# A fused attention, expert and MLP kernel: VectorE makes all tables of picks, ScalarE one product of the carry, and the MLP's step 1 is put in another order

## What is computed

```python
q_bucket, k_bucket = hash_of_signs(q @ proj), hash_of_signs(k @ proj)   # 6 bits
scores = where(q_bucket == k_bucket, q @ k.T / sqrt(64), -1e9)          # 2 x 8 heads, 768 x 768
x = softmax(scores) @ v                                                 # as rows: 1536 tokens x 512

logits = x @ w_gate + modality_bias[modality_id]                        # 8 experts
e = argmax(logits); gate = softmax(logits)[e]
y = gate * (relu(x @ w1[e]) @ w2[e])                                    # 512 -> 1024 -> 512

h = y @ w_in                                                            # 512 -> 2048
out = (maximum(h, 0) + log1p(exp(-abs(h)))) @ w_out                     # 2048 -> 512
```

## Time and profile before

| | us |
|---|---|
| median of 3 runs | 731.88 (731.85 to 732.01) |
| the profiled execution | 733.24 |
| its span, first to last instruction | 731.4 |
| attention and what comes ahead | 0 to 234.8 |
| dispatch | 234.8 to 272.1 |
| expert layers | 272.1 to 460.6 |
| MLP | 460.6 to 731.4 |

### The profile page before, as it was taken

One profiled execution on the slowest core, in us unless ns is written; L12 is line 12 of the kernel. 1 busy time (PEld: TensorE's weight loads), 2 busy tenths in 40 slices (PEclk: granted clock), 3 DMA queues, 4 the chain that ended last, 5 costly groups with the idle time before them and its releaser, 6 DMA issues. The chain is left out here.

```text
span 731.4 us, 13094 instructions
## 1 busy us (share of the span) xinstructions
PE 709.6 (97%) x4028; PEld 603.5 (83%) x4028; DVE 558.1 (76%) x897; ACT 489.1 (67%) x919; POOL 328.8 (45%) x303
## 2 busy tenths in 40 slices
PE   7999999999999979999999999999999999999996
PEld 4999999999998768888888878778887888878884
DVE  8999999989997556549991262598888788887874
ACT  7888888878887545459982464666566566566562
POOL 7987886788722710000000000255545845557543
PEclk9999999999999989999999999999999999999999
DMA  4215411132063483239990000133233423234221
GB/s 136 73 40 173 164 39 58 49 118 77 19 231 115 134 289 141 92 138 343 347 378 1 0 29 0 53 94 112 86 96 93 158 96 104 86 91 168 86 77 67
DMA packets 40530, 85.05 MB, mean 116 GB/s; under 512 B 5584, under 2 KB 9840, under 8 KB 40496
## 3 DMA queue, kind: packets, MB, share of 16 engines
q1 hardware_dynamic: 37776, 77.01, 31.2%
q0 software_dynamic: 2000, 6.98, 2.9%
q10 hardware_dynamic: 720, 0.64, 0.3%
HBM read 76.82 MB, written 6.68 MB: 114 GB/s over the span
## 5 line engine op out<-in xcount | busy, mean ns | idle before, releaser
L606 POOL TENSOR_TENSOR hres<-hexp,hres 128x512 f32<-128x512 f32 x46 | 60.0, 1305 | 306.7 <-DVE hres L1338 210.3
L678 ACT ACTIVATE pTh<-psA 128x384 fp32r<-128x384 f32 x192 | 83.8, 490 | 36.2 <-PE psA L1416 34.9
L966 DVE TENSOR_TENSOR pTl<-psA,pTh 128x384 fp32r<-128x384 f32 x192 | 97.9, 552 | 11.1 <-ACT pTh L678 9.7
L959 DVE TENSOR_SCALAR_CACHE_REDUCE psA<-psA 128x768 f32<-128x768 f32 x96 | 91.8, 956 | 1.7 <-PE psA L1410 1.6
L1410 PE MATMUL psA<-K,Q 128*128 128x384 f32 x384 | 89.9, 356 | 2.5 <-ACT probs L662 1.6
L662 ACT ACTIVATE probs<-psA,negmax 128x768 f32<-128x768 f32 x96 | 87.4, 911 | 0.4 <-DVE psA L959 0.4
L877 ACT ACTIVATE habs<-psA 128x512 f32<-128x512 f32 x48 | 28.7, 598 | 77.9 <-PE psA L1689 73.9
L1244 DVE TENSOR_TENSOR wil<-rawi,wih 128x512 fp32r<-128x512 f32 x48 | 77.5, 1617 | 0.0
L609 POOL TENSOR_TENSOR hsum<-hsum,hres 128x512 f32<-128x512 f32 x46 | 69.5, 1512 | 10.1 <-POOL hres L606 8.7
L1228 DVE SCALAR_TENSOR_TENSOR hTl<-psA,hTh 128x512 fp32r<-128x512 f32 x32 | 21.8, 685 | 67.5 <-ACT hTh L783 67.5
L1717 PE MATMUL psA<-woh,sl 128*128 128x512 f32 x180 | 70.2, 390 | 0.8 <-DVE sl L1317 0.8
(11 more groups left out here) (255 smaller groups left out, 1693.6 us busy)
## 6 DMA issues: line engine op xcount, KB each, us to landing
w2s<-in_moe_w SPq DMA_DIRECT2D x9, 2048.0 KB, 8.8
w1s<-in_moe_w SPq DMA_DIRECT2D x9, 2048.0 KB, 7.8
rawi<-in_moe_w_in SPq DMA_DIRECT2D x48, 256.0 KB, 2.7
rawo<-in_moe_w_out SPq DMA_DIRECT2D x48, 256.0 KB, 2.7
raw<-in_qk SPq DMA_DIRECT2D x16, 384.0 KB, 3.1
vs<-in_v SPq DMA_DIRECT2D x16, 192.0 KB, 2.4
x_rows<-X SPq DMA_DIRECT2D x1, 1728.0 KB, 6.5
x_rows<-X SPq DMA_DIRECT2D x1, 1512.0 KB, 5.5
```

The costliest lines, as they stand in the source:

```text
L678: nc.scalar.activation(pTh[u // TPGR % 2][:, g * TPH:(g + 1) * TPH, u % TPGR * P:(u % TPGR + 1) * P], psA[2][:, g, 0:HALF].rearrange("p (t ...
L959: V.tensor_scalar(psA[u % 2][:, :, 0:HALF], psA[u % 2][:, :, 0:HALF], PENALTY, PENALTY, ALU.min, ALU.min, accum_out=negmax[:, u % 4:u % 4 ...
L966: V.tensor_tensor(pTl[u // TPGR % 2][:, g * TPH:(g + 1) * TPH, cols], psA[2][:, g, 0:HALF].rearrange("p (t n) -> p t n", t=TPH), pTh[u // ...
```

## The change

In the dispatch VectorE makes all twelve tables of picks in two instructions of six, where it made ten in two of five; GpSimd's two are gone. ScalarE makes the carry's product with the row number, behind the exponential of the gates, and GpSimd keeps the other. On TensorE one group of the early first layer is done behind the 24 products and not ahead of them. In the MLP's step 1 VectorE makes its `hsum` ahead of `sl` of step 0, and the last expert tile is taken out of PSUM behind step 3, by ScalarE and by VectorE.

```diff
-PICKED = TILES - 2
...
             pool.tensor_tensor(carry[:, :, 0, :], within[:, :, :], over(iota_t[:, 0:TILES], TILES), ALU.mult).then_inc(carry_ready, 1)
-            pool.tensor_scalar(carry[:, :, 1, :], within[:, :, :], row_of[:, :], None, ALU.mult).then_inc(carry_ready, 1)
-            pool.wait_ge(lane_ready, 1)
-            for t in range(PICKED, TILES):
-                pool.tensor_scalar(pick[:, t, :], iota_p[:, :], lane_f[:, t:t + 1], None, ALU.is_equal).then_inc(carry_ready, 1)
...
             nc.scalar.activation(tmp8[:, :, :], tmp8[:, :, :], ACT.Exp).then_inc(gexp_done, 1)
+            act.wait_ge(consts, 12)
+            act.wait_ge(within_ready, 1)
+            nc.scalar.activation(carry[:, :, 1, :], within[:, :, :], ACT.Copy, scale=row_of[:, :]).then_inc(carry_ready, 1)
...
-                    if k == 1:
+                    if k == 3:
                         high_x2(final, nc.scalar.snap(col, min_val=0, max_val=B * S))
...
             for h in range(2):
-                ts = slice(h * PICKED // 2, (h + 1) * PICKED // 2)
-                V.tensor_tensor(pick[:, ts, :], iota_p[:, :].unsqueeze(1).broadcast_to([P, PICKED // 2, P]),
+                ts = slice(h * TPB, (h + 1) * TPB)
+                V.tensor_tensor(pick[:, ts, :], iota_p[:, :].unsqueeze(1).broadcast_to([P, TPB, P]),
                                 over(lane_f[:, ts], P), ALU.is_equal).then_inc(pick_ready, 1)
...
                     split_wo(k - 1, 1 - u)
-                    low(k - 1, 1 - u)
                     dve.wait_ge(l_done, k + 1)
                     V.scalar_tensor_tensor(hsum[u][:, :], hps[u], 0.0, hlog[u][:, :], ALU.max, ALU.add).then_inc(sum_done, 1)
+                    low(k - 1, 1 - u)
                     split_wi(k + LAG, u)
...
-                    if k == 1:
+                    if k == 3:
                         low_x2(final, nc.vector.snap(col, min_val=0, max_val=B * S))
...
-            first_layer(range(2, 6), w1s[1], xT0)
+            first_layer(range(2, 5), w1s[1], xT0)
...
-                if t < PICKED:
-                    pe.wait_ge(pick_ready, 1 + t // (PICKED // 2))
-                else:
-                    pe.wait_ge(carry_ready, 3 + t - PICKED)
+                pe.wait_ge(pick_ready, 1 + t // TPB)
...
-            first_layer(range(6, FC), w1s[1], xT0)
+            first_layer(range(5, FC), w1s[1], xT0)
```

## The result

| | before | after |
|---|---|---|
| median | 732.03 (731.61 to 733.43, 16 runs) | 730.38 (728.78 to 731.46, 16 runs) |
| span of the profiled execution | 731.4 | 729.4 |
| first gather starts | 243.41 | 242.26 |
| ScalarE and VectorE released | 260.74 to 260.80 | 259.56 to 259.62 |
| first turn of a layer row behind the gathered tiles (`yrow_bits`) | 271.70 | 270.42 |

A forecast was written before the change was run, and what follows sets the result against it. TensorE, busy 445.5 of 447.0 us from 272.05 us, was taken as the bound, so time saved earlier counts. Gathers and stall -1.3 us plus MLP -0.6 us give -1.9 us: 731.88 to 730.0 us, range 726.6 to 732.2 us.

The forecast's parts named there:

- Picks: Dispatch: VectorE's tables end at 240.5 to 240.7 us; `source` and the first gather come 1.3 us earlier, at 241.15 and 242.1 us.
- The product on ScalarE: Dispatch, carry's product: takes 0.3 us, 0.6 us at most; costs nothing, up to 0.3 us on hT.
- TensorE "has work queued until 257.4 us": Dispatch: TensorE stays busy until the stall, so earlier gathers by themselves do not speed it up before then.
- two signs of being wrong: Dispatch: TensorE running out before 257 us, or gathers lengthening once VectorE's gate chain overlaps them otherwise, would refute the forecast.
- rival 3: Dispatch: late signals start at an earlier turn and two more turns fall into the stall; +2.7 us, 734.6 us; chance 0.12.
- The stall: Dispatch, TensorE's 4.21 us gap: its end hangs on the gathers' end, so -1.3 us; bounds 0 and -1.3 us.
- The clock: Behind the stall, 1.2 GHz stretch: taken as unchanged, 0 us; bounds 0 and -2.8 us if the shorter gap keeps full clock.
- The MLP: Steps 1 to 3: earlier `hsum` cuts TensorE's step 3 wait, -0.6 us; x2h and x2l in step 3 cost nothing.
- Rival 4: MLP step 1: GpSimd takes the shared port first, TensorE waits 1.4 us for sl of step 0; 731.0 us; chance 0.06.
- Rival 2: Dispatch: the stall's end doesn't move, gathers not its cause; only the MLP's 0.6 us stays, 731.3 us; chance 0.17.
- rival 1: Dispatch: the shorter gap keeps the clock full, also -2.8 us, 727.2 us; chance 0.21.
- Rival 5: Dispatch: the stall vanishes, gathers running out before TensorE gets there; 4.2 + 2.8 + 0.6 gives 724.3 us; chance 0.07.

The follow-up runs named there:

- before_again: Kernel before, unaltered, run and traced once more in a place with late signals: 732.01 us, ratio 0.9994.
- mlp_only: Kernel before with only the MLP's edits, nothing of the dispatch: 731.77 us against 732.39 us, ratio 0.9995.
- dispatch_only: Changed kernel with the MLP's edits taken back: 730.07 us, ratio 0.9968 against the kernel before.
- after_again: Changed kernel, unaltered, run and traced once more in a place with late signals: 730.25 us, ratio 0.9970 against the kernel before.
- spare13: Changed kernel plus 13 matmuls on constants in TensorE's program ahead of the turn that waits in the stall: 730.32 us, ratio 0.9969 against the kernel before.
- extra3: Changed kernel plus three gathers into scratch tiles behind the twelve: 734.2 us, ratio 1.0027 against the kernel before.
- fourbuf_again: Changed kernel with four gated-row tiles and four PSUM turn buffers, not two: 727.74 us, ratio 0.9938; as fourbuf, without late signals, 723.58 us, 0.9981.
- throttle_again: Changed kernel with at most two gathers under way: 732.13 us, ratio 0.9991 against the kernel before at 732.72 us.
- group_ahead: Changed kernel with the early first layer's sixth group back ahead of the picks, in a place without late signals: 723.61 us, ratio 0.9979 against the kernel before.

## Why the prediction was right

The traces with late signals side by side (us; the release is VectorE's last one by such a signal, near the end of the gathers; "at 1.2 GHz" is the length of the stretch, wherever it starts):

| kernel | first gather | release | at 1.2 GHz | `yrow_bits` turn | from there to the end |
|---|---|---|---|---|---|
| before | 243.41 | 260.74 | 6.8 | 271.70 | 459.7 |
| before_again | 243.34 | 260.75 | 6.8 | 270.50 | 459.8 |
| mlp_only | 243.32 | 260.45 | 6.8 | 270.74 | 459.2 |
| dispatch_only | 241.93 | 259.13 | 3.4 | 268.90 | 459.8 |
| after | 242.26 | 259.56 | 6.8 | 270.42 | 459.0 |
| after_again | 242.34 | 259.53 | 3.4 | 270.23 | 459.0 |
| spare13 | 242.21 | 259.48 | 3.4 | 270.95 | 459.2 |
| extra3 | 242.26 | 263.66 | 10.2 | 274.37 | 459.3 |
| fourbuf_again | 242.00 | 259.43 | 0 | 266.70 | 459.2 |

- **Picks.** Right: tables end at 240.68 us (240.5 to 240.7 said), `source` 241.31 us (241.15), first gather 242.26 us (242.1). Of the 1.15 us the moved group gave about 0.35 us.
- **The product on ScalarE.** 0.40 us, between the 0.3 us taken and the bound of 0.6 us; it cost nothing.
- **TensorE "has work queued until 257.4 us".** This step failed. TensorE waits 1.19 us for the gates' sum, whose signal is held. It cost only 0.25 us at the stall's start, which is why the sum still held. The prediction gave two signs of being wrong, and both came: TensorE runs out before 257 us, and a gather is longer beside VectorE. It is also the first half of rival 3: the late signals do start earlier. Its second half, that more turns fall behind the stall, didn't happen here: the turn that waits is the same.
- **The stall.** Right in cause: the release follows the gathers' end, and extra3 moves it the other way. In size -1.18 us for -1.3 us, as the first gather moved by 1.15 us and not by 1.3 us. The reason given for it was not right: "issued at a fixed rhythm" fails, since of the 1.15 us at the first gather 0.81 us are left at the last. The release keeps its distance from the first gather (17.33 us before, 17.30 us after) and not from the last instruction, which ends 2.3 us ahead of it before (258.46 us) and 1.9 us after (257.65 us). Both repeats have the same releases to 0.03 us. What the prediction left open (why a signal is late) is now narrower: with three or more gathers under way, at the rate that they then have, TensorE is held.
- **The clock.** The value taken, 0, is what the two profiled executions show (6.8 us at 1.2 GHz in both, 0.7 and 0.9 us of it in the gap); before_again and after_again show that it could have come out otherwise, so this match is luck too. The reason given for the other bound was weak. The clock fell 1.9 us after TensorE ran out here and some 3.5 us after in the earlier trace rows, so a gap of 3.1 us was no protection, and a stretch of 3.4, 6.8 or 10.2 us followed in others. This term scatters by itself, some 1.7 us for 3.4 us more or less (at half the clock, work of that length loses half): the runs of the changed kernel lie 2.7 us apart. The gain itself is not the clock's: among executions with a mean granted clock of 0.993 the changed kernel's spans are 728.9 and 729.3 us, and those of the kernel before (beside mlp_only) 730.2 to 731.7 us; at 0.997 they are 727.0 to 729.1 us and 729.6 to 730.5 us.
- **The MLP.** -0.6 us said; 0.61 us less wait in the row, 459.0 to 459.3 us from the turn to the end in the six traces with the edit and 459.7 to 459.8 us in the three without it. The pair x2h and x2l stays hidden, as said.
- **The port.** Rival 4 is out: VectorE's `sl` ended at 469.41 us, 0.55 us behind GpSimd's `hres` (468.86 us), and not behind `hsum`, which ended at 470.56 us. The exclusive lock that the Trainium skill, "SBUF — State Buffer", section "SBUF: two separate sides", describes fits the row behind it: `wil` takes 1.78 us beside GpSimd's 1.52 us, and 0.68 us elsewhere.
- **Sum.** -1.3 - 0.6 = -1.9 us said. In the spans 731.4 - 729.4 = 2.0 us, in those of the repeats 730.3 - 729.2 = 1.1 us; in the medians 1.65 us, and 1.76 us between the repeats' (732.01 and 730.25 us).

Rival 2 (the release doesn't move) and rival 1 (the clock kept) didn't happen in the profiled execution. Rival 5, the stall gone, is what the place without the hold shows: 723.6 us for kernels like the changed one, where the rival's sum gave 724.3 us. But there the kernel before has lost its stall too, and the gain is not the stall's.

**Open.** Why some places have the hold and one did not, and by what path a backlog of gathers stops TensorE. One trait of the records goes with the place: each gather gives 16 landing events, and of the first eleven gathers the nine traces with late signals hold 0 to 9 events each, throttle_again 8 to 16, and the four traces of the other place all 16. That supports that throttle_again ran where the hold is. It also leaves a rival that no run tests: that the recording of the executions has a part in the hold.

Open is also how the 1.4 us of group_ahead come about without a stall to shorten; 0.6 us are the MLP's. For the rest there is a likely source. In group_ahead ScalarE's last tile is released by the last gather's landing and starts at 261.29 us, and TensorE waits for it:

```profile
262.07 0.54 PE L1414 MATMUL psA<-ident_r,xs_bits 128*128 128x128 f32 x4 [0.16 <-ACT xs L758]
```

So without the hold too the dispatch ends with the last gather, and gathers that come in earlier are worth something. How much isn't shown, since the kernel before wasn't traced there.

## What to carry to other kernels

Where two engines are released in the same 0.1 us by something the trace doesn't name, look at which traffic ends within half a microsecond of it, and move its end: here the stall moved along, whatever the rows call the releaser. An engine's signals that pass such a time should be few: four buffers instead of two, on top of the change, took away another 2.5 us (0.9938 for 0.9972, of 732 us), more than the change itself, at no cost in work. And price the clock as a draw: behind a gap that was shortened but not closed the slow stretch was 6.8 us long once and 3.4 us once. Where one trace of each kernel agrees with the forecast, take a second of each: the repeats here kept the release to 0.03 us and moved the turn behind it by 1.2 us.

## What the runs showed of the hardware

- With the gathers issued from GpSimd every 1.25 us, each some 3.9 us on the way, TensorE's signals acted up to 9.7 us late (extra3) in nine traces, and in six of them TensorE also started only one matmul in 0.7 to 2 us, from some 256 us on (extra3: 256.6 us and 258.7 us). With at most two under way, at 158 GB/s for 220 GB/s, nothing of the kind shows. The page "SBUF — State Buffer" of the Trainium skill, section "SBUF: two separate sides", says that a compute instruction can't be slowed by a DMA. For the matmuls themselves the rows agree, as far as modelled ends can tell: each is listed with its 0.27 us. What is held is their start and their signals.
- The hold belongs to where the kernel runs as much as to the kernel: the same code, fourbuf, takes 727.7 us with it and 723.6 us without, both traced. The kernel before takes 732 and 725 us.
- GpSimd's last gather instruction of the changed kernel ends at 257.65 us and the traffic 2.4 us later. The Trainium skill, "Perfetto Trace Analysis", section "DMA Instruction — SWDGE (GPSIMD)", says that such a row ends with the descriptors and not with the data; the trace agrees.
- The clock fell 1.9 us after TensorE ran out of work in the changed kernel, and in before_again at 258.3 us, 0.9 us after, where the kernel before kept it for 3.5 us with the same timeline. In after_again it fell at 259.0 us, when TensorE had been at work again for 1.4 us behind its gap of 3.40 us. The gap alone doesn't tell when.
